# Later steps for each couple of pairs in a fused Fourier mixer and feed-forward kernel

## The reference

```python
X = np.fft.rfft(x, axis=1)                      # 4 x 3008 x 256
Yr = Xr @ w_r - Xi @ w_i + b_r
Yi = Xr @ w_i + Xi @ w_r + b_i
Yr, Yi = (sign(Y) * maximum(abs(Y) - 0.01, 0) for Y in (Yr, Yi))
y = np.fft.irfft(Yr + 1j * Yi, n=3008, axis=1)
h = y.reshape(12032, 256) @ w_in                # 256 x 2048
g = maximum(h, 0) + alpha * minimum(h, 0)
out = g @ w_out                                 # 2048 x 256
```

## Time and profile before

| | |
|---|---|
| median of 3 runs | 1453.61 us (1453.17 to 1453.79) |
| the profiled execution's own time | 1453.01 us |
| its span, first to last instruction | 1451.2 us |
| PE busy | 1396.1 us (96%) |
| PEld busy | 1165.4 us (80%) |
| DVE busy | 945.8 us (65%) |
| ACT busy | 739.6 us (51%) |
| POOL busy | 311.1 us (21%) |
| mean granted TensorE clock | 0.995 |

### The profile page before, as it was taken

The page is one execution under the profiler, slowest core; times in us unless marked ns, Lnnn a source line. Parts: engine busy times, 40 slices in busy tenths (PEclk is TensorE's granted clock), DMA queues, the critical chain, the costliest instruction groups (busy, mean ns, idle before and its releaser), DMA issues. The chain is left out here.

```text
span 1451.2 us, 21472 instructions
## 1 busy us (share of the span) xinstructions
PE 1396.1 (96%) x7012; PEld 1165.4 (80%) x7012; DVE 945.8 (65%) x1824; ACT 739.6 (51%) x1646; POOL 311.1 (21%) x351
## 2 busy tenths in 40 slices
PE   7999999999999999999999999999999999999997
PEld 4987888878778888887788888888877888888886
DVE  5776777777755557777775556777776555555554
ACT  3775555555544545555554445555554444444443
POOL 0433532222201422222210242222220101001000
PEclk9999999999999999999999999999999999999999
DMA  6653522122110441212111142222210111011101
GB/s 217 193 149 125 159 56 69 52 66 62 46 38 14 133 107 51 66 57 66 53 35 38 53 119 73 61 62 61 62 44 21 31 26 26 16 22 31 21 15 15
DMA packets 163114, 94.68 MB, mean 65 GB/s; under 512 B 110500, under 2 KB 140628, under 8 KB 163004
## 3 DMA queue, kind: packets, MB, share of 16 engines
q1 hardware_dynamic: 158250, 88.91, 23.1%
q10 hardware_dynamic: 4754, 4.41, 1.0%
HBM read 55.74 MB, written 37.49 MB: 64 GB/s over the span
## 5 line engine op out<-in xcount | busy, mean ns | idle before, releaser
L1007 DVE SCALAR_TENSOR_TENSOR g_raw<-negpart,keep,h_ps 128x502 f32<-128x502 f32 (+1 forms) x384 | 282.5, 736 | 366.7 <-ACT negpart L785 363.9
L785 ACT ACTIVATE negpart<-h_ps 128x502 f32<-128x502 f32 (+1 forms) x384 | 224.5, 585 | 369.1 <-PE h_ps L461 368.8
L461 PE MATMUL out_ps<-g_hi,wout_hi 128*128 128x502 f32 (+1 forms) x768 | 313.1, 408 | 17.6 <-DVE g_lo L910 13.3
L461 PE MATMUL h_ps<-y_hi,win_hi 128*128 128x502 f32 (+1 forms) x768 | 300.7, 391 | 0.2 <-DVE y_lo L910 0.2
L461 PE MATMUL h_ps<-y_lo,win_hi 128*128 128x502 f32 (+1 forms) x768 | 300.6, 391 | 0.0
L461 PE MATMUL h_ps<-y_hi,win_lo 128*128 128x502 f32 (+1 forms) x768 | 299.5, 390 | 0.0
L461 PE MATMUL out_ps<-g_hi,wout_lo 128*128 128x502 f32 (+1 forms) x768 | 299.3, 390 | 0.0
L461 PE MATMUL out_ps<-g_lo,wout_hi 128*128 128x502 f32 (+1 forms) x768 | 298.5, 389 | 0.0
L910 DVE TENSOR_TENSOR g_lo<-g_raw,g_hi 128x502 fp32r<-128x502 f32 (+1 forms) x384 | 265.3, 691 | 0.1
L794 ACT ACTIVATE g_hi<-g_raw 128x502 fp32r<-128x502 f32 (+1 forms) x384 | 236.3, 615 | 0.3 <-DVE g_raw L1007 0.3
L461 PEld LDWEIGHTS out_ps<-g_hi,wout_hi 128*128 128x128 f32 x768 | 144.6, 188 | 52.3 <-DVE g_lo L910 23.2
(11 more groups left out here) (117 smaller groups left out, 2017.5 us busy)
## 6 DMA issues: line engine op xcount, KB each, us to landing
pair_raw<-fwd_scratch SPq DMA_DIRECT2D x96, 128.0 KB, 2.0
back_raw<-inv_scratch SPq DMA_DIRECT2D x61, 192.0 KB, 2.6
table<-in_twiddles_dram SPq DMA_DIRECT2D x28, 384.0 KB, 3.3
x_raw<-in_x_dram SPq DMA_DIRECT2D x64, 160.0 KB
inv_scratch<-inv_sb SPq DMA_DIRECT2D x36, 256.0 KB, 2.2
fwd_scratch<-staging SPq DMA_DIRECT2D x44, 192.0 KB, 2.1
out_dram<-turned SPq DMA_DIRECT2D x124, 40.0 KB, 2.0
inv_scratch<-inv_sb SPq DMA_DIRECT2D x24, 128.0 KB, 3.3
```

The lines of the kernel that those rows point to most:

```text
L461: mm = pe.matmul(ps, lhs, rhs, start=(first and n == 0), stop=(last and n == len(terms) - 1), **kw)
L785: act.activation(negpart[:, q % 2, 0:size], h_ps[:, q % 2, 0:size], ACT.Relu, scale=-1.0).then_inc(negpart_done, 1)
L1007: dve.scalar_tensor_tensor(g_raw[:, q % 2, 0:size], negpart[:, q % 2, 0:size], keep[:, m:m + 1], h_ps[:, q % 2, 0:size], ALU.mult, ALU.add ...
```

## The change

The steps of a couple are put further apart. Counted from the step of its odd pair: mixing and bias from +1 to +2, `above_couple`, threshold and split from +1 and +2 to +3, `rest_couple` from +2 to +4, the inverse and its copy from +4 to +5, the store from +5 to +6. In their steps, these functions are moved up to stand right behind the feed-forward's own work: on PE mixing comes ahead of `forward2`, on ACT `above_couple` ahead of `copy_more`, on DVE `rest_couple`, `shrink_couple` and `bias_couple` ahead of `whole_spec`. `split_couple` stays at the end of ACT's step. `split_whole` and `rest_whole` go behind the work on `y`. The high and low parts of the forward table are made two steps ahead of their first pair (before: four), those of the inverse table in its step (before: one ahead), and the next table is loaded a step later. The wait for `inv_copied` in `mix_couple` now stands ahead of the third part alone. No operation is added or taken away.

```diff
                     # SP
-                    p = p_unit(f, m, 1)
+                    p = p_unit(f, m, 2)
                     if p is not None and p % 3 == 0:
                         load_table(p // 3 + 1)
-                    p = p_couple(f, m, 5)
+                    p = p_couple(f, m, 6)
                     if p is not None:
                         store_couple(p)
...
                 pe.wait_ge(biased_done, p - 1)
-                if p % PAIRS == 1:
-                    pe.wait_ge(fwd_copied, S_HEAD * (p // PAIRS + 1))
-                else:
-                    pe.wait_ge(inv_copied, p - 1)
                 for ps, part, c in ((real_ps, 0, 1), (imag_ps, 1, 2), (sum_ps, 2, 0)):
                     if part == 2:
                         pe.wait_ge(sum_lo_done, p + 1 - PAIRS)
+                        if p % PAIRS == 1:
+                            pe.wait_ge(fwd_copied, S_HEAD * (p // PAIRS + 1))
+                        else:
+                            pe.wait_ge(inv_copied, p - 1)
...
                     # PE, behind hidden and forward1
+                    p = p_couple(f, m, 2)
+                    if p is not None:
+                        mix_couple(p)
                     p = p_unit(f, m, 0)
                     if p is not None:
                         forward2(p)
-                    p = p_couple(f, m, 4)
+                    p = p_couple(f, m, 5)
                     if p is not None:
                         inverse2(p - 1)
                         inverse2(p)
-                    p = p_couple(f, m, 1)
-                    if p is not None:
-                        mix_couple(p)
...
                     # ACT, behind bend and split_bent
+                    p = p_couple(f, m, 3)
+                    if p is not None:
+                        above_couple(p)
                     p = p_unit(f, m, 0)
                     if p is not None:
                         copy_more(p)
-                        split_whole(p)
+                    p = p_couple(f, m, 5)
+                    if p is not None:
+                        copy_couple(p)
                     u = i_unit(f, m)
                     if u is not None:
                         split_y(u)
-                    p = p_couple(f, m, 4)
-                    if p is not None:
-                        copy_couple(p)
+                    p = p_unit(f, m, 0)
+                    if p is not None:
+                        split_whole(p)
                     p = p_unit(f, m, -2)
                     if p is not None:
                         split_pair(p)
-                    p = p_unit(f, m, 0)
-                    if p is not None:
-                        split_sum(p)
                     v = i_bpair(f, m - 2)
                     if v is not None:
                         split_back(v)
...
-                    p = p_unit(f, m, -4)
+                    p = p_unit(f, m, -2)
                     if p is not None and p % 3 == 0:
                         split_tw(p // 3)
-                    p = p_unit(f, m, -1)
-                    if p is not None and p % 3 == 0:
-                        split_itw(p // 3)
-                    p = p_couple(f, m, 2)
+                    p = p_unit(f, m, 0)
+                    if p is not None:
+                        split_sum(p)
+                        if p % 3 == 0:
+                            split_itw(p // 3)
+                    p = p_couple(f, m, 3)
                     if p is not None:
                         split_couple(p)
-                    p = p_couple(f, m, 1)
-                    if p is not None:
-                        above_couple(p)
...
                     # DVE, behind bend, rest_bent, turn and split_x
+                    p = p_couple(f, m, 4)
+                    if p is not None:
+                        rest_couple(p)
+                    p = p_couple(f, m, 3)
+                    if p is not None:
+                        shrink_couple(p)
+                    p = p_couple(f, m, 2)
+                    if p is not None:
+                        bias_couple(p)
                     p = p_unit(f, m, 0)
                     if p is not None:
                         whole_spec(p)
-                        rest_whole(p)
                     u = i_unit(f, m)
                     if u is not None:
                         rest_y(u)
+                    p = p_unit(f, m, 0)
+                    if p is not None:
+                        rest_whole(p)
...
-                    p = p_couple(f, m, 2)
-                    if p is not None:
-                        shrink_couple(p)
                     p = p_unit(f, m, -2)
                     if p is not None:
                         rest_pair(p)
-                    p = p_couple(f, m, 2)
-                    if p is not None:
-                        rest_couple(p)
-                    p = p_couple(f, m, 1)
-                    if p is not None:
-                        bias_couple(p)
...
                     # POOL
-                    p = p_unit(f, m, -4)
+                    p = p_unit(f, m, -2)
                     if p is not None and p % 3 == 0:
                         rest_tw(p // 3)
-                    p = p_unit(f, m, -1)
+                    p = p_unit(f, m, 0)
                     if p is not None and p % 3 == 0:
                         rest_itw(p // 3)
```

## The result

The changed kernel takes 1444.94 us in the median of 7 runs (1442.37 to 1450.03), against 1453.79 us of the kernel before (7 runs, 1453.17 to 1454.39). The ratio is 0.9944, 95% interval 0.993 to 0.9958: 8.9 us won, where 33.6 were forecast. The runs of the changed kernel lie 7.7 us apart, those of before 1.2.

What follows compares the result with a forecast made beforehand. TensorE's stops were taken as the bound, 15.5 us in each of three stretches; 4.3 would stay and 11.2 go, 33.6 us in all, from 1453.01 to 1419.4, 1420.0 us as median. Forecast range 1410 to 1427, wider range 1410 to 1440.

Steps and rivals of the forecast that it cites:

- What bounds it: Tiles 1 to 4 of a batch: TensorE's stops set the end, 15.5 us per stretch; clock at its upper level.
- the tiles' starts: Start of every tile: idle time and a restart of 0.35 us stay, 1.1 us of a stretch's 15.5.
- Mixing a step later: Mixing at steps 2 and 6: all its 11 stops go, 8.4 us per stretch, with them stops ahead of an inverse.
- `above` and the bias: ScalarE takes `above` in the step after the bias without a wait; its 34.8 us of waiting per stretch go.
- Step 3: Threshold behind `above`; `split_couple` holds ScalarE, so step 4's `bend` is about 1.1 us late; called covered, no loss.
- steps 7 and 2: Fullest steps: step 7 leaves output products short, 1.4 us per stretch; step 2 nearly nothing, 0.3 us.
- the first steps of tile 3: VectorE's transposes of `turn` meet step 7's work and a table split: 1.2 us late and 0.3 restart, 1.5 us.
- The first: Rival: mixing stops go, output stops stay because ScalarE and VectorE remain late; 1430.5 us, chance 0.21.
- The port rival: GpSimd's SBUF reads make the `g_lo` behind each couple 0.85 us later; 1447.6 us, chance 0.07.
- three signs of being wrong: `bend` over 1.2 us late behind mixing; `g_lo` of 1.2 us or more behind couples; mixing's third part stopped for `inv_copied`.
- The clock: In tiles 1 to 4 it stands at 1.00, its upper level, 2.4 GHz, so nothing is to be had from it.

Runs made afterwards that it cites:

- late_couple: inv_behind_output with couple 11 of each batch taking above, threshold, splits, inverse, copy and store one step later: 1413.37 us.
- mix_a_step_earlier: Changed kernel with mixing on TensorE back at +1, behind the inverse, the bias still at +2: 1511.71 us.
- old_order_in_steps: inv_behind_output with the couple's work on ScalarE and VectorE back behind the pair's work within a step, at the changed steps: 1454.04 us.
- inv_behind_output: Changed kernel with a couple's two inverse products on TensorE behind their step's output product instead of ahead of it: 1420.22 us.
- short_pool: Changed kernel with GpSimd's passes over back_lo and the tables' low parts cut short, for measuring alone: 1440.11 us.
- short_pool_both: inv_behind_output and rest_a_step_earlier together, with GpSimd's passes cut as in short_pool, for measuring alone: 1418.21 us.
- rest_a_step_earlier: Changed kernel with rest_couple as VectorE's last piece of step +3 instead of its first at +4: 1420.64 us.
- pairs_a_step_earlier: inv_behind_output with all the pairs' work one step earlier against the tiles (21 for 22 in p_unit): 1427.72 us.

## Why the prediction was wrong, step by step

**What bounds it** held, but for the clock: TensorE's stops moved the time, and the 15.5 us of them in a stretch were sized about right. late_couple wins 245.9 - 232.1 = 13.8 us of them per stretch; with 1.1 for the tiles' starts that makes 14.9.

**Mixing a step later** held: no stop ahead of mixing is left. **`above` and the bias** held as well: ScalarE's ten long waits went. What I had not weighed is that these edits depend on each other: with the bias at +2 and mixing left at +1 the kernel loses (mix_a_step_earlier), and the steps without the order win nothing (old_order_in_steps).

**"Step 3" is where it failed, and with it the words "and with them stops ahead of an inverse" under "Mixing a step later".** I wrote that `split_couple` makes step 4's `bend` 1.1 us late, that this is "Covered", and that "Lateness of 1.5 in step 4 meets mixing at 6 and is gone". I asked for each late step only when the output product would need `g_lo`. The inverse products at 5 need `shr_lo`, which `rest_couple` makes behind `bend` and `g_lo` in that same late step 4, and they stand ahead of the output product in TensorE's step. The change had also brought the two nearer to each other, though it was to put the steps further apart: before, `rest_couple` at +2 and the inverse at +4, now +4 and +5. By the prediction's own numbers, for a couple A: the next `bend` on ScalarE 1.1 us late, so `g_lo` ends 2.16 + 1.1 = 3.3 us behind step 4's T and `shr_lo` 0.6 later, 3.9, where the inverse stands at 2.75 + 0.41 = 3.16: 0.7 us late. In the timeline above `g_lo` ends 218.55 - 215.24 = 3.31 behind T and `shr_lo` 3.90, with 0.70 us of idle time on TensorE: the prediction's lateness was right, only the wait that it met was missing. The nine stops measured 0.48 to 0.85. The sum had nothing for them and should have had 9.9 + 10 x 0.10 = 10.9 us per stretch. That this wait is the cause is shown twice over: moving the inverse behind the output product and moving `rest_couple` ahead each take the nine stops away and 24 us.

**The other terms.** With that one wait covered (inv_behind_output) the kernel takes 1420.2 us, the forecast's 1420.0; its stretch is 245.9 - 234.5 = 11.4 us shorter than before, against 11.2 forecast. The remainder is made up otherwise than I said: steps 7 and 2 leave almost nothing (forecast 1.4 and 0.3), the first steps of tile 3 more (a stop of 1.86 us and 1.3 for the clock, forecast 1.5). That the largest stop would be in tile 3 near m = 3 was foreseen. The agreement to a microsecond is thus partly luck.

**The rivals.** None was right. The first named a stay of the output stops, which went. The port rival has its mechanism, shown by short_pool and short_pool_both, and its 1447.6 is nearest to the 1444.9 measured, by accident: in the changed kernel the port costs 1444.9 - 1440.1 = 4.8 us, some 3 x 1.05 of it by `shr_lo` in tile 3 and 3 x 0.4 by held `g_lo` passes. Its price also had a slip: 11.2 - 9.7 leaves 1.5 won per stretch (1.8 with the 0.3 already counted), 1448 to 1449 us, not 2.0. None of the three signs of being wrong that I named would have pointed at `shr_lo`; the idle time did, 8.45 us in a stretch of 242.6 where 2 to 3.5 were to be. On "SBUF — State Buffer", section "Who interferes with whom", in the Trainium skill: by its rule a VectorE pass with two SBUF inputs that meets a running GpSimd pass that reads SBUF waits for its end. The trace agrees in who is held (`shr_lo` 1.76 us against 0.68); the held pass ended 0.56 us after POOL's (306.56 against 306.00), a little less than its own length of 0.68.

**The clock** was in none of my cases: "nothing is to be had from it" left out that there is something to lose, 1.3 us per fall. And the range, 1410 to 1440, rested on stops going or staying, with no room for one that comes.

## What to carry to other kernels

When a stage is moved by a step, write down for every product of TensorE which pass it waits for and when that pass runs in the new order, the moved ones too, not only for the product that stopped before, and see whether a pass and its product have come nearer to each other. Let a product whose result is not needed soon go last in its step: six matmuls moved by 1.38 us won 25 us here, nearly three times what the whole rescheduling had. And keep the step in which VectorE has most to do beside the step in which TensorE has most; parting them went with a loss of 67 us here, though its cause is argued and not shown.

## What the hardware showed that I had not expected

The granted clock fell to 0.50, the lower of its two levels, for 3.4 us behind stops of TensorE as short as 1.86 us (1.69 us of idle time, inv_behind_output), and behind two of 1.2 and 1.4 us close together. In late_couple, with no idle time over 0.6 us, it stayed at 1.00 from 130 to 1400 us. In between it is not decided by the stops alone. In the kernel before it stayed at 1.00 with 1.64 us of idle time, and the same stops can do either in one execution. In rest_a_step_earlier, tile 3 of each batch has idle times of 1.04 and 1.24 us with the same six matmuls between; the stretch behind them in batch 0 and in batch 1:

```profile
304.90:308.30 3.40, 3.40 (x17) 2.92 (x18) 2.43 (x5) 1.31 (x4) 0.99 (x2) 1.00 0.68 181
641.90:645.30 3.40, 3.37 (x8) 2.77 (x9) 2.42 (x5) 0.92 (x3) 0.99 (x2) 0.51 0.73 185
```

Likewise idle times of 1.90 us (short_pool_both) and 1.93 us (pairs_a_step_earlier) passed without a fall in batch 0 and were followed by one in batches 1 and 2. What decides was not tested further. In the changed kernel's profile the clock was down for 3.4, 3.4 and 6.8 us in the three batches. That may add to the spread of its runs, but the runs do not show it: the kernel before, which has no such fall in its profile, lay 4.5 us apart beside late_couple's 1.6.
